# Batched attention, gated FFN and routed experts: output product in step 1 of a pair, last batch written out, first FFN blocks between its last transposes and PV

## The reference

```
# attention: 4 batches, 8 heads, 576 positions, head size 64
scores = q @ k^T / 8       # masked where the key's block of 64 lies behind the query's
attn = exp(scores - rowmax);  attn /= rowsum + 1e-9;  o = attn @ v
# x: 2304 tokens x 512, the heads of a token side by side
y = (sigmoid(x @ w_gate) * (x @ w_val)) @ w_out         # 512 -> 1536 -> 512
# routing: each token goes to the one of 8 experts with the largest logit
out[t] = gate[t] * (relu(y[t] @ w1[e]) @ w2[e])         # 512 -> 1024 -> 512
```

## Time and profile before

| | us |
|---|---|
| median of 3 runs | 1006.93 |
| lowest and highest run | 1004.75, 1008.24 |
| the profiled execution's own time | 1004.57 |
| its span | 1002.8 |
| TensorE busy | 914.2 (91%) |
| Vector busy | 338.6 (34%) |
| ScalarE busy | 298.5 (30%) |
| GpSimd busy | 253.0 (25%) |

### The profile page before, as it was taken

One profiled execution on the slowest core, in us unless ns is written; L12 is line 12 of the kernel. 1 busy time (PEld: TensorE's weight loads), 2 busy tenths in 40 slices (PEclk: granted clock), 3 DMA queues, 4 the chain that ended last, 5 costly groups with the idle time before them and its releaser, 6 DMA issues.

```text
span 1002.8 us, 15746 instructions
## 1 busy us (share of the span) xinstructions
PE 914.2 (91%) x5370; PEld 758.2 (76%) x5371; DVE 338.6 (34%) x635; ACT 298.5 (30%) x654; POOL 253.0 (25%) x249
## 2 busy tenths in 40 slices
PE   7788777769999999999999999999388998999995
PEld 3444444438999999999999999999367887888884
DVE  5665666662121110120120120111744445235421
ACT  4443444542222122112111211211254344125310
POOL 4033333311121111111111111111253445225521
PEclk9999999999999999999999999999689999999998
DMA  4443444432220010010010000000374547115310
GB/s 130 136 150 107 137 140 147 134 117 89 74 63 32 1 32 32 1 32 13 21 32 1 32 1 1 32 1 1 118 267 160 184 155 258 42 42 209 120 42 30
DMA packets 45536, 83.08 MB, mean 83 GB/s; under 512 B 6831, under 2 KB 19119, under 8 KB 45488
## 3 DMA queue, kind: packets, MB, share of 16 engines
q1 hardware_dynamic: 39728, 67.21, 20.8%
q0 software_dynamic: 3360, 10.49, 3.2%
q10 hardware_dynamic: 2400, 4.72, 1.2%
HBM read 68.17 MB, written 14.75 MB: 83 GB/s over the span
## 4 chain that ended last, share of the span: by engine, by line
PE 70%; POOL 2%; issue 2%; DMA 1%; DVE 1%; ACT 0%; POOLq 0%; ACTq 0%; SPq 0%; DVEq 0%
PE bank L1162 21%; PE bank L1163 21%; PE bank L1164 21%; PE bank L1299 2%; PE bank L1221 1%; DMA stage<-in_we 1%; POOL ew1l L368 1%; PE bank L1212 1%; PE bank L1273 1%; POOL ew2l L368 0%; PE bank L1129 0%; PE bank L1264 0%; POOL yg L598 0%; POOL out L615 0%; POOL ag L587 0%
## 5 line engine op out<-in xcount | busy, mean ns | idle before, releaser
L1162 PE MATMUL bank<-xh,w1h 128*128 128x384 f32 x576 | 196.1, 340 | 0.0
L1164 PE MATMUL bank<-xh,w1l 128*128 128x384 f32 x576 | 193.3, 336 | 0.0
L1163 PE MATMUL bank<-xl,w1h 128*128 128x384 f32 x576 | 193.2, 335 | 0.0
L573 POOL TENSOR_TENSOR hl<-hraw,hh 128x384 fp32r<-128x384 f32 x72 | 77.1, 1071 | 406.5 <-ACT hh L701 406.5
L889 DVE TENSOR_TENSOR hraw<-sig,bank 128x384 f32<-128x384 f32 x72 | 39.9, 554 | 349.2 <-ACT sig L730 349.2
L730 ACT ACTIVATE sig<-bank 128x384 f32<-128x384 f32 x72 | 35.4, 492 | 262.6 <-PE bank L1164 262.6
L672 ACT ACTIVATE prob<-bank,nmax 128x576 f32<-128x576 f32 (+2 forms) x144 | 76.1, 529 | 118.1 <-DVE nmax L842 112.9
L1162 PEld LDWEIGHTS bank<-xh,w1h 128*128 128x128 f32 x576 | 108.3, 188 | 1.8
L1163 PEld LDWEIGHTS bank<-xl,w1h 128*128 128x128 f32 x576 | 108.3, 188 | 1.7
L1164 PEld LDWEIGHTS bank<-xh,w1l 128*128 128x128 f32 x576 | 108.1, 188 | 0.0
L1090 PE MATMUL bank<-kt,qt 64*64 64x64 f32 (+7 forms) x640 | 71.7, 441 | 15.6 <-ACT prob L672 10.3
(11 more groups left out here) (147 smaller groups left out, 1306.8 us busy)
## 6 DMA issues: line engine op xcount, KB each, us to landing
stage<-in_we SPq DMA_DIRECT2D x56, 512.0 KB, 4.4
w1raw<-in_w SPq DMA_DIRECT2D x8, 768.0 KB, 5.5
kt<-in_kT SPq DMA_DIRECT2D x16, 288.0 KB, 3.7
qt<-in_qT SPq DMA_DIRECT2D x16, 288.0 KB, 4.2
rwide<-rinv_scratch SPq DMA_DIRECT2D x32, 144.0 KB, 3.1
xt_scratch<-xo SPq DMA_DIRECT2D x16, 288.0 KB, 2.1
xraw<-xt_scratch SPq DMA_DIRECT2D x6, 768.0 KB, 4.7
y_scratch<-yrow ACTq DMA_DIRECT2D x6, 768.0 KB, 3.6
```

What stands on the lines that cost most here:

```text
L573: pool.tensor_tensor(hl[:, f % 2, :], hraw[:, f % 2, :], hh[:, f % 2, :].bitcast(F32), ALU.subtract).then_inc(h_low, 1)
L1162: pe.matmul(out_, wh, ah, start=first, stop=False, skip_group_check=True)
L1163: pe.matmul(out_, wh, al, start=False, stop=False, skip_group_check=True)
L1164: return pe.matmul(out_, wl, ah, start=False, stop=last, skip_group_check=True)
```

## The change

The output product moves from step 3 to step 1 of a pair, and on SP the store of `xo` goes ahead of the reciprocals' store. The loop over batches ends one batch earlier on all engines, and the last batch is written out. The first x block is loaded before the last batch; GpSimd splits it (`x_split`) in that batch, behind the kt scaling of p = 1. Behind the last pair TensorE does two transposing steps, the first `up` block, the other two transposing steps, PV, the second `up` block. Vector does the last `recips` between its last copies, `o_out` of pair 14 behind them, and `o_out` of pair 15 after the first `hraw`. SP loads w_out as soon as PV is done, and stores the last `xo` in front of w_out's third block. `woraw` moves in the layout, off the `xo` buffers.

```diff
@@ -122,9 +122,9 @@
         hl = sb(s2, "hl", [P, 2, GT], F32R)
         woh = sb(s2, "woh", [P, FC, D], F32R)
         wol = sb(s2, "wol", [P, FC, D], F32R)
+        woraw = sb(s2, "woraw", [P, 2, D])
         xh.append(sb(s2, "xh1", [P, C, GT], F32R))
         xl.append(sb(s2, "xl1", [P, C, GT], F32R))
-        woraw = sb(s2, "woraw", [P, 2, D])
         yrow = sb(s2, "yrow", [P, GM, D])
         yT = sb(s2, "yT", [P, C, P])
         s2.close()
@@ -306,7 +306,7 @@
         W1_STEP = 4
 
         PV_STEP = {4: [0], 6: [1, 2, 3, 4]}
-        RSUM_STEP, O_STEP = 2, 3
+        RSUM_STEP, O_STEP = 2, 1
 
         def evac_pT(copy, p, j, u, t0, t1, done):
 
@@ -428,11 +428,11 @@
                 sp.dma_start(kt[p % 2][:], qkv_at(kT, g)).then_inc(qk_loaded[p % 2], 16)
                 sp.dma_start(qt[p % 2][:], qkv_at(qT, g)).then_inc(qk_loaded[p % 2], 16)
                 if not early:
-                    rinv_store(g - 2, p % 2)
                     if p == 3:
                         o_store(b, 0)
-                    elif not isinstance(b, int):
+                    elif not (isinstance(b, int) and b == 0):
                         o_store(b - 1, p + 1)
+                    rinv_store(g - 2, p % 2)
                     rwide_load(g - 2, p % 2)
                     sp.wait_ge(pv_done, g - 1)
                 sp.dma_start(vt[p % 2][:, 0:KT_N - 1, :],
@@ -450,10 +450,9 @@
             for p in range(PPB):
                 pair(0, p)
             sp.dma_start(wr_sb[:], wr.rearrange("(c p) e -> p c e", p=P)).then_inc(wr_loaded, 16)
-            with sp.Fori(1, BATCH) as b:
+            with sp.Fori(1, BATCH - 1) as b:
                 for p in range(PPB):
                     pair(b, p)
-
 
             def xload(G, pairs_stored):
                 for i in range(2):
@@ -465,18 +464,19 @@
                              ).then_inc(x_loaded, 16)
 
             xload(0, PPB)
+            for p in range(PPB):
+                pair(BATCH - 1, p)
+            o_store(BATCH - 1, PPB - 3)
             rinv_store(NPAIR - 2, 0)
-            o_store(BATCH - 1, PPB - 3)
             rwide_load(NPAIR - 2, 0)
+            o_store(BATCH - 1, PPB - 2)
             rinv_store(NPAIR - 1, 1)
-            o_store(BATCH - 1, PPB - 2)
             rwide_load(NPAIR - 1, 1)
-            o_store(BATCH - 1, PPB - 1)
             sp.wait_ge(pv_done, NPAIR)
-            sp.wait_ge(w1_low, 2 * C)
-            for i in range(2):
-                sp.wait_ge(xo_stored[i], 16 * NPAIR // 2)
+            sp.wait_ge(scores_done, NB * NPAIR)
             for k in range(FC):
+                if k == 2:
+                    o_store(BATCH - 1, PPB - 1)
                 if k >= 2:
                     sp.wait_ge(wo_high, k - 1)
                     sp.wait_ge(wo_low, k - 1)
@@ -546,6 +546,16 @@
                                    w1h[:, bass.ds(k, 1), :].rearrange("p a f -> p (a f)").bitcast(F32),
                                    ALU.subtract).then_inc(w1_low, 1)
 
+            def x_split():
+
+                pool.wait_ge(x_loaded, 16)
+                pool.tensor_copy(xh[0][:].rearrange("p c n -> p (c n)"), xraw[:].rearrange("p c n -> p (c n)")
+                                 ).then_inc(x_high, 1)
+                pool.wait_ge(x_high, 1)
+                pool.tensor_tensor(xl[0][:].rearrange("p c n -> p (c n)"), xraw[:].rearrange("p c n -> p (c n)"),
+                                   xh[0][:].rearrange("p c n -> p (c n)").bitcast(F32), ALU.subtract
+                                   ).then_inc(x_low, 1)
+
             def pair(b, p):
                 g = b * PPB + p
                 if not (isinstance(g, int) and g == 0):
@@ -555,14 +565,18 @@
 
                 if p == 2:
                     w1_split(2 * b)
-                elif p == 0 and not isinstance(b, int):
+                elif p == 0 and not (isinstance(b, int) and b == 0):
                     w1_split(2 * b - 1)
+                elif p == 1 and isinstance(b, int) and b == BATCH - 1:
+                    x_split()
 
             for p in range(PPB):
                 pair(0, p)
-            with pool.Fori(1, BATCH) as b:
+            with pool.Fori(1, BATCH - 1) as b:
                 for p in range(PPB):
                     pair(b, p)
+            for p in range(PPB):
+                pair(BATCH - 1, p)
             w1_split(2 * C - 1)
 
             def hlow(G, f):
@@ -679,9 +693,11 @@
 
             for p in range(PPB):
                 pair(0, p)
-            with act.Fori(1, BATCH) as b:
+            with act.Fori(1, BATCH - 1) as b:
                 for p in range(PPB):
                     pair(b, p)
+            for p in range(PPB):
+                pair(BATCH - 1, p)
 
             def xhigh(G, par):
                 act.wait_ge(x_loaded, 16 * (G + 1))
@@ -690,7 +706,6 @@
 
             for i in range(NB - LAG, NB):
                 after_unit(NPAIR - 1, 1, i)
-            xhigh(0, 0)
             act.wait_ge(scores_done, NB * NPAIR)
             act.wait_ge(w1_low, 2 * C)
 
@@ -852,20 +867,21 @@
 
             for p in range(PPB):
                 pair(0, p)
-            with dve.Fori(1, BATCH) as b:
+            with dve.Fori(1, BATCH - 1) as b:
                 for p in range(PPB):
                     pair(b, p)
-            recips(NPAIR - 1, 1)
+            for p in range(PPB):
+                pair(BATCH - 1, p)
 
             def xlow(G, par):
                 dve.wait_ge(x_high, G + 1)
                 dve.tensor_tensor(xl[par][:], xraw[:], xh[par][:].bitcast(F32), ALU.subtract).then_inc(x_low, 1)
 
-            for i in range(NB - LAG, NB):
-                after_unit(NPAIR - 1, 1, i)
-            xlow(0, 0)
+            after_unit(NPAIR - 1, 1, NB - LAG)
+            after_unit(NPAIR - 1, 1, NB - LAG + 1)
+            recips(NPAIR - 1, 1)
+            after_unit(NPAIR - 1, 1, NB - 1)
             o_out(NPAIR - 2, 0)
-            o_out(NPAIR - 1, 1)
 
             def yT_evac(i, m, last=False):
                 dve.wait_ge(yT_done, i + 1)
@@ -887,6 +903,8 @@
                         dve.wait_ge(h_high, n - 1)
                         dve.wait_ge(h_low, n - 1)
                     dve.tensor_tensor(hraw[:, f % 2, :], sig[:, f % 2, :], val_ps, ALU.mult).then_inc(hraw_done, 1)
+                    if first and f == 0:
+                        o_out(NPAIR - 1, 1)
                     if first:
                         dve.wait_ge(wo_high, f + 1)
                         dve.tensor_tensor(wol[:, f, :], woraw[:, f % 2, :], woh[:, f, :].bitcast(F32),
@@ -1147,16 +1165,11 @@
 
             for p in range(PPB):
                 pair(0, p)
-            with pe.Fori(1, BATCH) as b:
+            with pe.Fori(1, BATCH - 1) as b:
                 for p in range(PPB):
                     pair(b, p)
-            for i in range(NB - PE_LAG, NB):
-                turn(NPAIR - 1, PPB - 1, i)
-            pv(NPAIR - 1, PPB - 1, list(range(KT_N)))
-
-
-            pe.wait_ge(exp_done, NB * NPAIR)
-
+            for p in range(PPB):
+                pair(BATCH - 1, p)
             def three(out_, wh, wl, ah, al, first, last):
 
                 pe.matmul(out_, wh, ah, start=first, stop=False, skip_group_check=True)
@@ -1225,7 +1238,8 @@
             def group(G, par):
                 first = isinstance(G, int) and G == 0
                 for f in range(FC):
-                    up(G, par, f)
+                    if not (first and f < 2):
+                        up(G, par, f)
                     if f >= 2:
                         down(G, f - 2)
                     elif not first:
@@ -1236,6 +1250,15 @@
                         if f in LG_STEP:
                             router(GM * (G - 1) + LG_STEP.index(f), LG_STEP.index(f))
 
+            turn(NPAIR - 1, PPB - 1, NB - 4)
+            turn(NPAIR - 1, PPB - 1, NB - 3)
+            pe.wait_ge(exp_done, NB * NPAIR - 2)
+            up(0, 0, 0)
+            turn(NPAIR - 1, PPB - 1, NB - 2)
+            turn(NPAIR - 1, PPB - 1, NB - 1)
+            pv(NPAIR - 1, PPB - 1, list(range(KT_N)))
+            pe.wait_ge(exp_done, NB * NPAIR)
+            up(0, 0, 1)
             group(0, 0)
             group(1, 1)
             with pe.Fori(1, NG // 2 - 1) as k:
```

## The result

The changed kernel takes 993.45 us as the median of 4 runs (988.32 to 996.92), the kernel before 1006.99 (4 runs, 1004.75 to 1008.24). The ratio is 0.9864, with a 95% interval from 0.9830 to 0.9899: faster by 1.4%, or 13.5 us of the 15.3 forecast. The profiled execution took 996.28 us, its span is 994.6, so it is one of the two longer of the four.

The account below looks back on a forecast made before the run. The prediction took TensorE's attention waits as the bound, above all PV waiting for Vector's output product (30.0 us in 15 waits). Its terms, 10.7 + 4.6 = 15.3 us off the 1006.93 median, gave 991.6, range 986.5 to 998.

Parts of the forecast that it names:

- Part 1: Attention pairs 2 to 15: product in step 1 wins 0.82 us each, 11.5, less 0.8 for GpSimd's hold: 10.7 us.
- the chain from the exponential to PV: In each pair: ScalarE's exponential, copy, TensorE's transpose of unit 1, then PV; 1.26 us, taken from pair 1.
- the exponential's start: In pair 15: ScalarE's exponential starts at about 210.76 instead of 209.69, after step 2's reduction ends at 210.72.
- The hold by GpSimd: Reciprocals' tensor_scalar on Vector, seven even pairs: held some 1.0 us by GpSimd's kt scaling, costing 0.8 us in all.
- Rival C: GpSimd's hold lasts the whole kt scaling, 1.65 us; seven pairs lose 5.3 us instead of 0.8: 996.1, chance 0.12.
- Part 2: x split and load, loops, SP order: x work leaves the attention's end; the last batch outside the loop gives nothing.
- The x split on GpSimd: GpSimd's cast (1.46 us) and subtraction (3.45 us) stand behind a kt scaling; 4.9 us are covered by its later wait.
- Part 3: End of the attention: third up block starts 4.6 us earlier; 2.9 if idle time before PV drops the clock.
- Rival D: Pairs: clock stays at the upper level in all; pairs 2 and 6 give back 2.7 us: 988.9, chance 0.13.
- rival E: Idle time in one piece drops the clock in every pair, 12 more falls, and at the end: 1009.5, chance 0.03.
- B: Rival: the wait only moves, the later exponential keeps PV in place, only part 3 counts: 1002.3, chance 0.08.
- F: Rival: PV doesn't wait for the product, or loads are late, and nothing changes: 1007, chance 0.02.

Follow-up runs that it names:

- experiment 1: Kernel before with only the output product moved from step 3 to step 1: 997.29 us, ratio 0.9931.
- experiment 6: Changed kernel with five filler matmuls (result unused) in the wait ahead of unit 1's transpose, from the third pair on: 989.22 us, ratio 0.9821.
- experiment 7: Changed kernel with five fillers ahead of unit 1 and, at the end, pair 14's product ahead of Vector's last transposes' copy: 986.11 us, ratio 0.9795.
- experiment 10: Changed kernel with all 16 pairs written out, five fillers ahead of unit 1, and pair 14's product ahead of Vector's last copies: 985.58 us, ratio 0.9777.
- experiment 2: Changed kernel with the output product put back in step 3: 1003.63 us, ratio 0.9964.
- experiment 8: Changed kernel with all 16 pairs written out and pair 14's product ahead of Vector's last copies, no fillers: 987.66 us, ratio 0.9811.
- experiment 5: Changed kernel run again without edit, in the second job: 991.30 us, ratio 0.9861.
- experiment 3: Changed kernel with the last reciprocals and pair 14's product ahead of Vector's last transposes' copy at the end: 990.51 us, ratio 0.9854.
- experiment 9: Changed kernel with the first up block moved from between the last transposes to behind the last PV: 991.51 us, ratio 0.9844.
- experiment 4: Changed kernel with ten filler matmuls in the wait ahead of unit 1's transpose, from the third pair on: 999.45 us, ratio 0.9936.
- experiment 11: Changed kernel with five fillers behind unit 1's transpose, in front of PV's first part, the wait left empty: 1010.95 us, ratio 1.0030.

## Why the prediction was right, and where its sizes were off

The direction, the mechanism and the range held; 991.6 was forecast, 993.45 and 991.30 were measured in two jobs.

**Part 1, size too large.** "0.82 us are won" per pair is 0.60 to 0.63 in a loop (experiment 1; 0.51 in pairs 4, 8 and 12, the first of each batch) and 0.68 for pairs written out both before and after (pair 3: 13.33 before, 12.65 now). Two steps failed. The first is the chain from the exponential to PV, which I took from pair 1 as 1.26 us. In pair 5 it is 72.23 - 70.83 = 1.40, part of it at the lower clock; in pair 10, looped and without a fall, it is 141.16 - 139.79 = 1.37:

```profile
139.79 0.63 ACT L686 ACTIVATE prob<-bank,nmax 128x448 f32<-128x448 f32 x1 [1.10 <-DVE nmax L857]
...
141.16 1.19 PE L1147 MATMUL bank<-pt,vt 128*64 128x320 f32 x8
```

The second is the exponential's start. I let it follow the reduction by 0.04 us, where the earlier trace rows has 209.69 - 209.57 = 0.12; moved by the same 1.15 us as the reduction it would have been 210.84, 3.79 us into the pair, and 3.79 or 3.80 is what looped pairs show. The two, 0.11 and 0.08 us, are the difference between 0.82 and the measured 0.63. Pair 1 is written out, the pairs it was applied to are looped. In the changed kernel's written-out pair 3 the chain is 46.34 - 45.05 = 1.29, near the forecast:

```profile
45.05 0.63 ACT L686 ACTIVATE prob<-bank,nmax 128x448 f32<-128x448 f32 x1 [1.08 <-DVE nmax L857]
...
46.08 0.30 PE L1120 MATMUL bank<-ident,prob 128*128 128x128 f32 x1 [1.35 <-ACT pt L316]
...
46.34 1.19 PE L1147 MATMUL bank<-pt,vt 128*64 128x320 f32 x8
```

**The hold by GpSimd cost next to nothing.** I forecast about 1.0 us of hold in seven pairs and 0.8 us of loss. The rows of pair 8, where both start together, and pair 15 of experiment 6, where w1's cast is the neighbour:

```profile
112.23 1.65 POOL L564 TENSOR_SCALAR kt<-kt 128x576 f32<-128x576 f32 x1 [4.63 <-DMA qt<-in_qT]
112.28 0.64 DVE L820 TENSOR_SCALAR rsum<-rsum 128x9 f32<-128x9 f32 x1
```

```profile
198.62 1.46 POOL L543 CAST w1h<-w1raw 128x1536 fp32r<-128x1536 f32 x1 [11.71 <-DMA w1raw<-in_w]
198.81 1.30 DVE L820 TENSOR_SCALAR rsum<-rsum 128x9 f32<-128x9 f32 x1
```

Behind the kt scaling the tensor_scalar is held for about 0.5 us and ends at 112.92, while the scaling runs on to 113.88. Behind the cast it is held to its end, 200.11 against 200.08, as in the earlier trace rows. In the changed kernel's seven even pairs only three show a hold, of 0.13 to 0.48 us, and each of the three ends 0.68 or 0.69 us after the scaling's start. In pair 10 the tensor_scalar starts 0.60 us behind the scaling, with 1.05 us of it still to run, and takes 0.17 us as if alone. One hold ran on to the scaling's end all the same: pair 10 of experiment 7, 0.53 us, done at 135.05 against 135.02. The held pairs are at most 0.1 us longer than the same pairs of experiment 1 (pair 6: 12.98 against 12.88). Even a hold of over a microsecond costs little: pair 15 up to the reciprocals takes 12.66 us in experiment 7 (held, 1.44 us) and 12.46 in experiment 10 (not held, 0.17). Rival C is out. The contention that the Trainium skill names in "GPSIMD Engine Reference", Key points, is seen here, in a Vector instruction with one SBUF input; no trace shows its perf mode. The length isn't in that section. Here it depends on GpSimd's operation, and what I made of it, a hold to the end of any instruction, is wrong.

**Part 2, an edit costed at nothing that gives.** "The last batch ... issues the same instructions on each engine: nothing" is the second step that failed. Writing out takes 0.17 us off a pair before the change and about 0.22 after it (experiments 2 and 8). Pairs 12 to 15 gain some 0.8 us from that, which by chance makes up for part of the too large 0.82. I had seen the 13.33 us of pair 3 before and did not use it:

```profile
43.90:57.23 13.33, 10.76 (x101) 5.89 (x105) 8.60 (x22) 6.23 (x22) 6.50 (x3) 1.00 0.53 168
```

The x split on GpSimd was covered as forecast: cast and subtraction of 1.47 and 3.45 us ran in pair 12, and the next kt scaling still waited 8.8 us for its load (4.9 us had been forecast as covered).

**Part 3, the lower of my two values.** I took 4.6 us, since the clock would stay up for PV behind a dense up block, and named 2.9 for the other case. Measured are 2.86. The wait for the product was as forecast (2.31 us, 2.5 forecast); the clock fell behind it all the same, in spite of the dense block ahead. That is the step with the largest error, 1.7 us. The first down block had no wait, as forecast.

**Luck in the sum.** In the profile of experiment 5 the stretch from pair 2 to the last transposes is 180.3 us (28.21 to 208.52) against 191.2 before, and the end, to the third up block, 16.2 (to 224.71) against 19.0. With the falls taken out (one here, two before, some 1.5 us each), the pairs are worth 9.4 us and the end 2.8: 12.2, where 10.7 + 4.6 = 15.3 were forecast. The medians came out 13.5 and 15.2 us below the kernel before, nearer to the forecast than the terms. The likely reason is the clock: its mean is 0.970 to 0.972 in most runs of the kernel before and 0.975 to 0.978 in six of the ten of the changed one, a gain that the prediction had put at nothing. So the mechanism was right, and part of the closeness of the number is chance.

**The clock in pairs.** Rival D (fewer falls) and rival E (more) both named it. The profiles without fillers inside the wait, and with the product in step 1 at the old amount of work, have none (experiment 1), one (3, 5, 8 and 9) and four falls in pairs (the first), against two in the kernel before and two in experiment 2. So D was right for the fastest runs (988.32 and 989.08 against its 988.9), and E in a small part for the slowest: two falls more, not twelve. The idle time ahead of PV shrank from 0.34 + 1.82 us to 1.5, but it is now one piece. Experiments 4, 6, 7, 10 and 11 show that what TensorE does inside that piece decides. Why some pairs fall and their neighbours with the same rows don't stays open, and so does whether one piece is worse than two of the same sum, which no run tried.

B and F are out by the first experiment.

## What to carry to other kernels

When a stall for an engine is removed by moving that engine's work earlier, follow what now stands behind the moved work: here 0.6 of 1.8 us arrived, and the rest became a wait at another place. A block put into a wait fills it only if the work that the wait is for doesn't itself stand behind that block; look at the order on the other engine first. Where the clock falls in a regular wait, cheap filler work that fits into the wait can pay for itself.

## What was not expected of the hardware

- Added work made the kernel faster: five unused matmuls in each of fourteen waits (1.35 us each) took the median from 991.30 to 989.22 us and the spread from 7.6 to 1.6 us, in one job. The same five behind the wait cost 20 us (1010.95).
- The granted clock fell to 1.2 GHz after TensorE had idled 1.5 us in a pair (0.91 in that microsecond, 0.50 in the three that followed), and 1.1 us into the PV that followed 2.3 us of idle time behind 4.2 us of dense matmuls at the end of the attention. With 0.56 us of idle time there (experiment 3) it stayed up.
- The same instructions take 0.17 to 0.22 us per pair longer in a loop than written out. The cause was not tested.
- A small Vector tensor_scalar between SBUF buffers is held by GpSimd's cast up to its end (1.30 us instead of 0.16), but by GpSimd's tensor_scalar on kt (1.65 us) only for up to 0.5 us: with one exception in experiment 7, the held instruction ended 0.7 us after the scaling's start.
